# Delta-rule attention stage of a three-stage kernel: chain products over the whole array, keys turned by full transposes, a stage without loops, and N block-diagonal over two heads

## What is computed

```python
def _attn_ref(q, k, v, beta):            # B, H, S, D = 4, 8, 768, 48
    k_n = k / (np.linalg.norm(k, axis=-1, keepdims=True) + 1e-06)
    state = np.zeros((B, H, D, D))
    for t in range(S):
        kt, vt, bt = (k_n[:, :, t], v[:, :, t], beta[:, :, t, None])
        y[:, :, t] = np.einsum('bhd,bhde->bhe', q[:, :, t], state)
        v_old = np.einsum('bhde,bhd->bhe', state, kt)
        state = state + bt[:, :, :, None] * np.einsum('bhd,bhe->bhde', kt, vt - v_old)
```

## Time and profile before

| | |
|---|---|
| median of 3 runs | 1244.67 us (1233.08 to 1247.83) |
| the profiled execution | 1252.97 us, span 1251.3 us |
| PE, PEld busy | 1025.1 us (82%), 907.0 us (72%) |
| DVE, ACT, POOL busy | 477.0, 326.4, 338.1 us |
| instruction queue, q8 | 122 packets, 2.00 MB |

### The profile page before, as it was taken

The page is one execution under the profiler, slowest core; times in us unless marked ns, Lnnn a source line. Parts: engine busy times, 40 slices in busy tenths (PEclk is TensorE's granted clock), DMA queues, the critical chain, the costliest instruction groups (busy, mean ns, idle before and its releaser), DMA issues. The chain is left out here.

```text
span 1251.3 us, 38030 instructions
## 1 busy us (share of the span) xinstructions
PE 1025.1 (82%) x16548; PEld 907.0 (72%) x16549; DVE 477.0 (38%) x890; ACT 326.4 (26%) x636; POOL 338.1 (27%) x226
## 2 busy tenths in 40 slices
PE   2688888868868888850598889899959999999999
PEld 2677777767767877740487778787848888888888
DVE  1345454544435454442233343333324232232311
ACT  0334333434323343310121221212212121221211
POOL 3332233223403321118505544415531010000000
PEclk9989998989979899875799999999979999999999
DMA  8501111110111110005323423333320101100000
GB/s 295 217 19 50 36 32 36 48 37 19 50 35 35 33 33 18 3 3 193 119 103 132 138 78 108 127 128 113 113 60 29 32 20 44 31 25 26 1 26 26
DMA packets 34455, 83.51 MB, mean 67 GB/s; under 512 B 4240, under 2 KB 23184, under 8 KB 31760
## 3 DMA queue, kind: packets, MB, share of 16 engines
q1 hardware_dynamic: 28656, 45.22, 11.0%
q0 software_dynamic: 5664, 36.18, 8.7%
HBM read 58.58 MB, written 22.81 MB: 65 GB/s over the span
## 5 line engine op out<-in xcount | busy, mean ns | idle before, releaser
L1011 PE MATMUL hb<-early,last_h 128*128 128x512 f32 x648 | 204.8, 398 | 4.7 <-ACT o_sb L1125 3.6
L1011 PEld LDWEIGHTS hb<-early,last_h 128*128 128x128 f32 x648 | 121.1, 190 | 31.0 <-ACT o_sb L1125 2.7
L1011 PE MATMUL hb<-early,last_l 128*128 128x512 f32 x324 | 127.5, 393 | 0.0
L299 PEld LDWEIGHTS bank<-t,n_hi 64*64 64x64 f16 x2688 | 75.8, 114 | 22.3 <-issue 11.4
L299 PE MATMUL bank<-t,n_hi 64*64 64x64 f16 x2688 | 79.1, 198 | 11.5 <-issue 10.4
L456 ACT CAST t<-bank 128x512 f16<-128x512 f32 x96 | 56.3, 587 | 119.4 <-PE bank L299 117.8
L497 DVE TENSOR_TENSOR p<-bank,cf 128x512 f16<-128x512 f32 x96 | 66.0, 688 | 42.8 <-PE bank L299 41.9
L587 POOL COPY x_all<-y_tile 128x384 f32<-128x384 f32 (+1 forms) x24 | 12.5, 521 | 257.0 <-DVE y_tile L513 257.0
L933 POOL TENSOR_TENSOR late<-w_raw,late 128x3072 fp32r<-128x3072 f32 x8 | 59.7, 7457 | 71.5 <-DVE late L920 71.4
L1149 DVE TENSOR_TENSOR m<-hb,m 128x512 f32<-128x512 f32 x36 | 24.9, 692 | 132.8 <-PE hb L1011 132.8
L1011 PE MATMUL ob<-wo_h,early 128*128 128x384 f32 x288 | 74.2, 335 | 0.0
(11 more groups left out here) (154 smaller groups left out, 2271.6 us busy)
## 6 DMA issues: line engine op xcount, KB each, us to landing
w_raw<-w POOLq DMA_DIRECT2D x14, 1536.0 KB, 7.2
k_raw<-kh SPq DMA_DIRECT2D x24, 256.0 KB, 4.9
kq_t<-qh SPq DMA_DIRECT2D x24, 256.0 KB, 2.8
x_sorted<-zeros SPq DMA_DIRECT2D x32, 192.0 KB, 2.2
x_in<-x_sorted SPq DMA_DIRECT2D x29, 192.0 KB, 2.4
y_sorted<-y_sb SPq DMA_DIRECT2D x28, 192.0 KB, 1.9
v_in<-vh SPq DMA_DIRECT2D x24, 192.0 KB, 2.8
out<-o_sb SPq DMA_DIRECT2D x24, 192.0 KB, 1.9
```

Of the source, the lines that this page charges most:

```text
L299: ins = pe.matmul(out[s, C * u:C * u + C], lhs(s, u), rhs(s, u), start=first and u == 0, stop=True, skip_group_check=True)
L1011: ins = pe.matmul(out, a[x], b[y], start=first and i == 0, stop=last and i == 2, skip_group_check=True)
```

## The change

- K', the chain's products, and the products of N on the left are done with the whole array. The state, rhs and z of a pair of heads are stored block-diagonal (each [P, NP, 2, D], zero outside a head's own half), and so is n_hi. One "ks" product with K' and Q side by side as 128 weight columns gives K'S in the partitions 0 to 63 and QS in 64 to 127, "z" has 64 weight columns, and "up" has K beta and A as 128. So "ks", "z", "up" are 4 calls each in place of 8, 8 and 24, with 96 columns in place of 48. A dummy product of 8 columns goes ahead of "up".
- The keys are loaded twice, one time by chunk in the partitions for the transposes (kt_in), and one time as before, now called k_own, for K beta. "kt" is 4 transposes of 128x128.
- DVE scales beta by the norms (beta_k, four small operations per step); POOL multiplies k_own by it. POOL also waits more often for its own last result.
- The outputs are copied by ACT, 64x384 at a time, in place of two DVE copies; the rhs, z, n_hi, n_lo and state operations are cut in two by head. The reset by a mask is gone; a memset is there once per sequence.
- update, turn, gram, the residue's n_lo part and the last inverse products stay on quarters.
- No loop is left in the stage; all 12 steps are written out on each engine.
- Q is stored interleaved with K' in kq_t, in pieces of 64 floats. DVE writes zeros to the new arrays first (some 20 memsets), and PE, ACT and POOL wait for that.

```diff
-    kh = np.pad(k.reshape(shape).transpose(g, s, st, hh, t, e, p, d), pad).reshape(TILES, P, U, DP)
+    k, v, beta = k.reshape(shape), v.reshape(shape), beta.reshape(shape[:-1])
+    kt = k.transpose(g, s, st, e, t, p, hh, d).reshape(TILES, P, U, D)
+    kh = k.transpose(g, s, st, hh, t, e, p, d).reshape(TILES, P, U, D)
     qh = np.pad(q.reshape(shape).transpose(g, s, st, hh, e, p, t, d), pad).transpose(0, 1, 2, 3, 7, 4, 5, 6)
-    vh = v.reshape(shape).transpose(g, s, st, hh, t, e, p, d).reshape(TILES, P, 2, NP, D)
-    bh = beta.reshape(shape[:-1]).transpose(hh, t, g, s, st, e, p).reshape(P, TILES, U)
-    return [np.ascontiguousarray(a) for a in (kh, qh.reshape(TILES, P, U, C), vh, bh)]
+    vh = v.transpose(g, s, st, hh, t, e, p, d).reshape(TILES, P, 2, NP, D)
+    bh = np.stack([beta.transpose(hh, t, g, s, st, e, p).reshape(P, TILES, U),
+                   beta.transpose(e, t, g, s, st, p, hh).reshape(P, TILES, U)], axis=1)
+    return [np.ascontiguousarray(a) for a in (kt, kh, qh.reshape(TILES, P, U, C), vh, bh)]
...
-    n_p = double("n_p", [P, U, 2, C], F32)
+    n_kb_a = double("n_kb_a", [P, U, 3, C], F32)
...
-    def run(eng, body):
-
-        def walk_of(w):
-            def of(k):
-                return step(k // 2, k % 2) if 0 <= k < STEPS else None
-            body(of(w), of(w - 1), of(w - 2), of(w + 1))
-        for w in range(-1, 4):
-            walk_of(w)
-        with eng.Fori(2, STEPS // 2 - 1) as m:
-            body(step(m, 0), step(m - 1, 1), step(m - 1, 0), step(m, 1))
-            body(step(m, 1), step(m, 0), step(m - 1, 1), step(m + 1, 0))
-        for w in range(STEPS - 2, STEPS + 2):
-            walk_of(w)
+    def run(body):
+
+        for w in range(-1, STEPS + 2):
+            body(*(k if 0 <= k < STEPS else None for k in (w, w - 1, w - 2, w + 1)))
...
-        def load_k(k, m, par):
+        def load_k(k, par):
             for st in range(2):
-                if not before(k, 2):
+                if k >= 2:
                     sp.wait_ge(kn_ready[st], k - 1)
-                sp.dma_start(k_raw[par][:, st], kh[2 * k + st]).then_inc(k_in[par][st], 16)
-
-        def load_qv(k, m, par):
+                sp.dma_start(k_raw[par][:, st], kt_in[2 * k + st]).then_inc(k_in[par], 16)
             for st in range(2):
-                if not before(k, 2):
+                if k >= 2:
+                    sp.wait_ge(kb_ready[st], k - 1)
+                sp.dma_start(k_own[par][st][:], kh[2 * k + st]).then_inc(k_own_in[par], 16)
+
+        def load_qv(k, par):
+            for st in range(2):
+                if k >= 2:
                     sp.wait_ge(state_out[st], 2 * k - 2)
-                sp.dma_start(kq_t[par][st][:, 1], qh[2 * k + st]).then_inc(q_in[par][st], 16)
-                sp.dma_start(v_in[par][st][:], vh[2 * k + st]).then_inc(v_got[par][st], 16)
-        load_k(*step(0, 0))
+                sp.dma_start(kq_t[par][st][:, :, 1, :], qh[2 * k + st]).then_inc(qv_in[par][st], 16)
+                sp.dma_start(v_in[par][st][:], vh[2 * k + st]).then_inc(qv_in[par][st], 16)
...
+        load_k(2, 0)
+        for k in range(2, STEPS):
+            if k + 1 < STEPS:
+                load_k(k + 1, (k + 1) % 2)
+            load_qv(k, k % 2)
...
+        def both_heads(lhs, rhs, out, first=False):
+
+            for u in range(U):
+                ins = pe.matmul(out[:, C * u:C * u + C], lhs[:, u].rearrange("q h c -> q (h c)"), rhs(u), start=first and u == 0,
+                                stop=True, skip_group_check=True)
+            return ins
+
+        def whole(lhs, rhs, out, first):
+
+            return pe.matmul(out[:, :], lhs, rhs, start=first, stop=True, skip_group_check=True)
...
-                for u in range(U):
-                    for s in half:
-                        ins = pe.matmul(tb[s, C * u:C * u + C], kn[par][st][s, u, :], ident[s, s], start=u == 0, stop=True,
-                                        skip_group_check=True)
+                for p in range(NP):
+                    ins = pe.transpose(tb[:, P * p:P * p + P], kn[par][st][:, 2 * p:2 * p + 2, :].rearrange("q h d -> q (h d)"), ident)
...
-                diagonal(ident16, ident_rep, pb, True)
-                each_head(n, eye if lv == 0 else t, pb).then_inc(jacobi_done[st], 1)
+                whole(ident16, ident_rep, pb, True)
+                both_heads(n, lambda u: ident_rep[:, 0:C] if lv == 0 else t16[st][:, u, :], pb).then_inc(jacobi_done[st], 1)
...
-                each_head(n, t, pb, first=True).then_inc(prod_done[st], 1)
+                both_heads(n, lambda u: t16[st][:, u, :], pb, first=True).then_inc(prod_done[st], 1)
...
-                diagonal(ident16, ident_rep, pb, True)
-                diagonal(neg16, flat(t16[st]), pb, False)
-                each_head(n, t, pb)
+                whole(ident16, ident_rep, pb, True)
+                whole(neg16, flat(t16[st]), pb, False)
+                both_heads(n, lambda u: t16[st][:, u, :], pb)
...
                 pe.sem_inc(passed_pe, 1)
                 for p in range(NP):
-                    for s, r in zip(half, rows):
-                        ins = pe.matmul(out[s, W + D * p:W + D * p + D], kq[r, 0, NP * e + p, :], state[st][r, p, :],
-                                        start=p == 0, stop=True, skip_group_check=True)
+                    ins = pe.matmul(out[:, W * p:W * p + W], kq_t[par][st][:, NP * e + p, :, :].rearrange("q a t -> q (a t)"),
+                                    state[st][:, p].rearrange("q h d -> q (h d)"), start=p == 0, stop=True, skip_group_check=True)
                 ins.then_inc(ks_done[st], 1)
             elif what == "z":
-                pe.wait_ge(rhs_out[st], 2 * k + e + 1)
+                pe.wait_ge(rhs_out[st], 4 * k + 2 * e + 2)
                 if e == 0:
                     pe.wait_ge(inv_out[st], k + 1)
                 pe.sem_inc(passed_pe, 1)
                 for p in range(NP):
-                    for s in half:
-                        ins = pe.matmul(out[s, W + D * p:W + D * p + D], t_inv[st][s, NP * e + p, :], rhs[st][s, p, :],
-                                        start=p == 0, stop=True, skip_group_check=True)
+                    ins = pe.matmul(out[0:C, W * p:W * p + W], t_inv[st][:, NP * e + p, :], rhs[st][:, p].rearrange("q h d -> q (h d)"),
+                                    start=p == 0, stop=True, skip_group_check=True)
                 ins.then_inc(z_done[st], 1)
             elif what == "up":
-                pe.wait_ge(z_out[st], 2 * k + e + 1)
+                pe.wait_ge(z_out[st], 4 * k + 2 * e + 2)
                 if e == 0:
                     pe.wait_ge(kb_ready[st], k + 1)
                 pe.sem_inc(passed_pe, 1)
+                pe.matmul(out[0:C, X:X + 8], ident16[:, 0:C], ident16[:, 0:8], start=True, stop=True, skip_group_check=True)
                 for p in range(NP):
-                    for s, r in zip(half, rows):
-                        pe.matmul(out[s, D * p:D * p + D], kq[r, 1, NP * e + p, :], state[st][r, p, :], start=p == 0, stop=False,
-                                  skip_group_check=True)
-                for p in range(NP):
-                    for s in half:
-                        pe.matmul(out[s, D * p:D * p + D], n_p[par][st][s, NP * e + p, 1, :], z[st][s, p, :], start=False, stop=True,
-                                  skip_group_check=True)
-                for p in range(NP):
-                    for s in half:
-                        ins = pe.matmul(out[s, W + D * p:W + D * p + D], kb[par][st][s, NP * e + p, :], z[st][s, p, :],
-                                        start=False, stop=True, skip_group_check=True)
+                    ins = pe.matmul(out[:, W * p:W * p + W], n_kb_a[par][st][:, NP * e + p, 1:3, :].rearrange("q a t -> q (a t)"),
+                                    z[st][:, p].rearrange("q h d -> q (h d)"), start=False, stop=True, skip_group_check=True)
                 ins.then_inc(up_done[st], 1)
...
             elif what == "split":
-                act.copy(n_hi[st][:], n_p[par][st][:, :, 0, :]).then_inc(n_hi_ready[st], 1)
+                for hh, s in enumerate(half):
+                    act.copy(n_hi[st][s, :, hh, :], n_kb_a[par][st][s, :, 0, :]).then_inc(n_hi_ready[st], 1)
...
-                act.copy(z[st][:].rearrange("p n d -> p (n d)"), yb[st][:, W:2 * W]).then_inc(z_out[st], 1)
+                for hh in range(2):
+                    act.copy(z[st][half[hh], :, hh, :], by_head[0:C, hh]).then_inc(z_out[st], 1)
+            elif what == "up":
+                act.wait_ge(up_done[st], 2 * k + e + 1)
+                if e == 0 and k >= 1:
+                    act.wait_ge(x_out[st], k)
+                act.copy(y_tile[st][half[e], :], yb[st][C:P, 0:X]).then_inc(y_out[st], 1)
...
                 if e == 0:
-                    dve.wait_ge(v_got[par][st], 16 * m + 16)
-                dve.tensor_tensor(rhs[st][:], v_in[par][st][:, e], yb[st][:, W:2 * W].rearrange("p (n d) -> p n d", n=NP),
```

(39 more changed lines are left out.)

192 lines of the change are left out of this document (104 added, 88 removed).

## The result

| | median | profiled execution | span | stage ends |
|---|---|---|---|---|
| before | 1242.2 us (1233.08 to 1247.83, 4 runs) | 1252.97 us | 1251.3 us | 550.57 us |
| changed | 1315.16 us (1313.74 to 1319.0, 4 runs) | 1313.74 us | 1312.1 us | 612.84 us |

The ratio is 1.06, with a 95% interval of 1.0529 to 1.067: slower, where 1225 us and the range of 1192 to 1263 were forecast. "Stage ends" is the start of the last copy of router logits on DVE; what follows takes 700 us in both. The loss of 61 us between the two spans lies in the attention stage. Between the medians it is 73 us: a fourth run of the kernel before has been added to the three known at the prediction, and its profiled execution lies 11 us above the median.

A forecast was written before the change was run, and what follows sets the result against it. TensorE was taken to bound the attention stage. Terms -12 + 5 + 0 + 30 - 43 - 12 + 6 + 2 + 4 = -20 us took 1252.97 profiled to 1233, a median of about 1225 us; range 1192 to 1263.

The forecast's parts named there:

- Evictions: Copies and splits on DVE and ACT: DVE about even, ACT 2.4 us more per pair, charged 6 us in all.
- SP and POOL: K's loads on SP also wait for POOL's K beta, ahead of Q and V: charged 2 us in all.
- signs of being wrong: Gram or its next product waiting for DMA, issue rows above 30 us, clock below 0.9, N's products far from 0.25 us.
- Issue: TensorE's idle time with no cause shown, 51.4 us in ten steps: fewer instructions leave 8, so 43 us less.
- stalls stay: Rival: issue time not set by instruction count, only the two loop pieces (13 us) go; 1261 us, chance 0.2.
- Switches: TensorE changing between quarters and whole array: 262 more at 0.15 us, 30 us charged; 128x128 to 128x64 taken as 0.
- Key transposes: Quarter products become four full 128-column transposes per step and stream: 0.96 us falls to 0.45, 12 us less.
- Chain: Whole-array chain products, 0.88 us per 128x128 and 0.67 for z: 2.46 us per half step for 2.35, 5 us more.
- N's products: 16 quarter calls become 8 full ones with N block-diagonal: 0.25 us as now, taken as 0, upper bound 21 us more.
- Clock: Lower TensorE clock in the ten steps costs 21 us; 12 given back, clock row 0.96 or more if right.
- Q late: Rival: POOL's K beta holds SP, SP holds Q, gram waits, 5 us per step; 1287 us, chance 0.1.
- cheap array: Rival: the 128-column f32 load is hidden and most switches fall into waits; 1198 us, chance 0.2.

The follow-up runs named there:

- e1_two_beta_k: The changed kernel with two beta_k buffers instead of one, DVE waiting for K beta of step k - 1: 1204.2 us, ratio to before 0.9674.
- e4_before_unrolled: The kernel before with all 12 steps of the attention stage written out and no other edit: 1212.77 us, ratio to before 0.9758.
- e5_dummy_at_z: e1_two_beta_k with the dummy product issued at the end of z instead of ahead of up: 1201.91 us, ratio to before 0.9634.
- e7_more_switches: e1_two_beta_k with the identity part of each jacobi product on quarters, 551 switches for 468: 1206.38 us, ratio to before 0.9664.
- e12_n_in_one: e9_only_kt_full with n_hi stored as before the change, and n_hi and n_lo made by one operation each, not two: 1225.57 us, ratio to before 0.9785.
- e8_chain_on_quarters: e1_two_beta_k with the chain's products on quarters as before the change, N's products still whole: 1200.27 us, ratio to before 0.9625.
- e10_slot12: The changed kernel, one beta_k buffer, with DVE's scaling of beta in slot 12 instead of slot 10: 1269.97 us, ratio to before 1.0135.
- e9_only_kt_full: e8_chain_on_quarters with N's products on quarters too, only the key transposes staying whole: 1241.19 us, ratio to before 0.9895.

## Why the prediction was wrong

**The wait.** The step that failed is in "Evictions" and "SP and POOL": the scaling of beta to beta_k on DVE, listed among the parts of the change, is in no term of the sum, and its wait on kb_ready was not followed. Both were thus put at nothing without a reason. The prediction did follow kb_ready for SP, where it cost nothing (in the changed kernel Q lands after 3.1 us and no product waits for it), and missed the same semaphore on DVE, where its row now reads 90.4 us, with 77.7 us of standing on TensorE and the clock's fall after it. It wrote out POOL's work from x_all to K beta for SP's sake, and never asked which other engine stands still until then. Two buffers give all of it back, 111 us. Of the signs of being wrong two came: issue rows above 30 us (77.7 in one row) and a clock below 0.9 (0.88). Without this wait the change gives 1204 us, inside the range and 21 below the forecast; so the remaining terms are judged on e1_two_beta_k, whose window is

```profile
92.00:500.00 408.00, 373.31 (x7619) 321.46 (x7617) 212.91 (x485) 221.19 (x460) 137.94 (x131) 1.00 0.15 41
```

The 21 us come mostly from two terms, as an estimate from what follows: at 4.5 us for 154 switches the 372 new ones cost 11 us, not 30, and the clock gave back 21 us, not 12. That is 28 us; other terms were too small, so that the sum came within 21 us is in part luck.

**Issue.** 43 of 51.4 us were to go and rows below 15 to stay. With all such rows of TensorE from 92 to 500 us added, 19.9 us stay in e1_two_beta_k, of 59.8 before: nearly right, though not below 15. Its source was half right. The loop pieces were priced at 13 us; the written-out stage alone is worth 30 us by the ratio (39 between the stage ends, but the profiled execution of before lay above its median), with 37.4 us of issue rows left. The rival "stalls stay" had 1261 us and falls with e1_two_beta_k. The Trainium skill, Runtime: NRT & Kernel Launch, section Instruction fetch mechanics, says that a taken branch breaks the sequential prefetch of instructions. e4_before_unrolled has no loop in the stage and keeps 37.4 us at 11896 records in 408 us, e1_two_beta_k 19.9 at 7619. So if these pieces are waits for instructions, which no row names, they do not hang on branches alone.

**Switches.** The prediction took 0.15 us each from two of them in the kernel before; the rows now show 0.10, and the 110 between 128x128 and 128x64 are not free. The timeline of e1_two_beta_k, and then that of e5_dummy_at_z, at full clock:

```profile
303.33 0.40 PE L296 MATMUL bank<-t,n_hi 128*128 128x64 f16 x8
303.65 0.44 PE L283 MATMUL bank<-ch,t 64*64 64x64 f16 x16
303.93 0.42 PE L283 MATMUL bank<-tt,p 64*64 64x64 f16 x16
304.27 0.88 PE L395 MATMUL chain<-rhs,t_inv 128*64 128x96 f32 x8
305.08 0.44 PE L283 MATMUL bank<-p,tt 64*64 64x64 f16 x16
305.35 0.42 PE L283 MATMUL bank<-tt,p 64*64 64x64 f16 x16
305.70 0.66 PE L318 MATMUL bank<-cf,kn 128*128 128x128 f32 x4
306.19 1.03 PE L386 MATMUL chain<-state,kq_t 128*128 128x96 f32 x8
307.06 0.40 PE L296 MATMUL bank<-t,n_hi 128*128 128x64 f16 x8
...
311.26 0.87 PE L395 MATMUL chain<-rhs,t_inv 128*64 128x96 f32 x8
312.07 0.41 PE L296 MATMUL bank<-t,n_hi 128*128 128x64 f16 x8
```

```profile
308.48 0.87 PE L395 MATMUL chain<-rhs,t_inv 128*64 128x96 f32 x8
309.19 0.17 PE L397 MATMUL chain<-ch 128*64 128x8 f16 x1
```

From z to quarters it is 0.81 us (304.27 to 305.08), from z to a 128x128 product the same 0.81 (311.26 to 312.07), and to a product in its own 128x64 form 0.71: 0.10 us for each kind of switch. From 92 to 492 us it is 0.80 or 0.81 in all 10 and 11 places of the first two kinds, and 0.68 to 0.72 in 44 of the last. The Trainium skill, TensorEngine Tiling (Array Packing), section Key Properties, says that a change of tiling mode drains TensorE; the trace agrees for this kind too, and my zero was wrong. What was mis-sized is the share that lies on TensorE's path: 30 us were charged, and between e5_dummy_at_z and e7_more_switches 154 switches go with 4.5 us. That most of them fall where TensorE would have waited for DVE or ACT is likely and not shown.

**Products.** Key transposes: 0.49 us (305.70 to 306.19) for 0.45, right; that this is worth 12 us in the whole no run shows (e12_n_in_one has them and is no faster than e4_before_unrolled). Chain: 0.87 us for eight records of 128x96 (306.19 to 307.06) against 0.88, and z 0.71 against 0.67, right. Its worth of 5 us more can't be read alone: e8_chain_on_quarters, which takes back the chain with its 110 switches and adds 1296 calls, is 4 us faster than e1_two_beta_k (6 by the ratios), within the scatter. N's products: a single one does cost the same (303.33 to 303.65, 0.32 us with its switch), but their worth of 0 was wrong, 11 to 34 us by the ratios, most of it in issue rows and clock; the sum had the fewer instructions under "issue" only.

**Evictions.** 6 us were charged for all of them. e12_n_in_one shows 14 us for the split of n_hi and n_lo alone, in a kernel with N and the chain on quarters; what it costs in e1_two_beta_k was not tested.

**Clock, start.** 1.00 in e1_two_beta_k, above the 0.96 that would show it right: all of the 21 us came back, where 12 were taken. In the changed kernel it is 0.88, with the lower level after each wait. Start: POOL's first squares move from 14.85 to 18.43 us, 3.6 for 4, right.

**The rivals.** The one on the slow side was "Q late", a wait in order behind POOL's K beta. It was of the right kind, with the clock's fall after it, but it had the wrong engine (SP, not DVE) and 5 us per step, not 8. Of "cheap array" the hidden switches came true and the cheaper chain did not.

## What to carry to other kernels

For every wait that a change adds, follow the semaphore to its writer, write down what that writer stands behind on its own engine and in which slot this is made, and compare it with the slot of the waiter; if it comes later, the waiter's whole engine stands. A second buffer or a slot late enough takes the wait away; here both gave the same time, and one slot behind the obvious place (slot 12) was not enough. When TensorE waits for "issue" at a product that has a semaphore wait, look for another engine that stands at the same moment. And judge a rewrite by its parts: here most of the gain was to be had from the written-out loop, 30 us, and the whole-array chain, the part with most code in it, brought nothing once N's products were on the whole array.

## What the hardware showed beside it

- A wait of TensorE of 7.7 us was followed by nearly 7 us at 1.2 GHz, one of 4.2 us by 3.2 us. In these two steps the clock adds some 40% to the price of the wait.
- DVE's four operations on 64x8 took 2.88 us together behind the long wait (2.88 in e10_slot12 too) and 0.68 us in e1_two_beta_k, where POOL is idle; behind the wait POOL scales kn and makes beta_mask (344.00 to 346.69) at the same time. That POOL's work slows them was not tested.
- TensorE's idle time without a cause in the profile from 92 to 500 us is 37.4 us without a loop at 29 matmul records per us and 19.9 us at 19 per us, but 22.2 at 25 in e8_chain_on_quarters and 45.8 at 26 in e9_only_kt_full: the rate alone does not set it. What else does is open.
